# The down projection of layer 2 by rows of tokens: hidden activations stationary, weights moving

## The reference, cut to what matters

```
kv   = einsum('bhsd,bhse->bhde', k, v)
out  = einsum('bhsd,bhde->bhse', q, kv)
x    = (out / rms(out) * g_norm)         # as 4608 x 512
h    = sigmoid(x @ w_gate) * (x @ w_val)     # layer 1, 512 -> 1536
x    = h @ w_out                             # 1536 -> 512
g    = x @ w2_gate
h    = g * sigmoid(g) * (x @ w2_val)         # layer 2
out  = h @ w2_out                            # 4608 x 512, float32
```

## Time and profile before

| | us |
|---|---|
| median of 3 runs | 1740.79 (1740.44 to 1740.86) |
| profiled execution, its own time | 1741.19 |
| its span | 1738.8 |
| PE busy | 1717.6 (99%) |
| DVE busy | 1204.9 (69%) |
| ACT busy | 890.0 (51%) |
| POOL busy | 376.1 (22%) |

### The profile page before, as it was taken

How to read it: one execution, slowest core, us unless ns; L and a number is a source line. 1 busy time by engine, 2 the same in 40 slices (tenths; PEclk the granted TensorE clock), 3 DMA queues, 4 the chain that set the end, 5 groups by cost and what they waited for, 6 DMA issues and landing times.

```text
span 1738.8 us, 30846 instructions
## 1 busy us (share of the span) xinstructions
PE 1717.6 (99%) x11190; PEld 1686.7 (97%) x11190; DVE 1204.9 (69%) x1938; ACT 890.0 (51%) x1709; POOL 376.1 (22%) x326
## 2 busy tenths in 40 slices
PE   8899999999999999999999999999999999999998
PEld 7899999999999999999999999999999999999998
DVE  4876677787666678666679877787666668655556
ACT  5666666555444445444456555555444445444444
POOL 5822222013111125111136000013111124111111
PEclk9999999999999999999999999999999999999999
DMA  9887887586555567555556555576555566555553
GB/s 232 252 264 209 277 254 211 211 298 229 200 200 200 200 222 250 197 198 199 195 188 216 195 198 199 199 250 241 201 198 197 200 220 238 167 180 186 184 187 97
DMA packets 200150, 366.91 MB, mean 211 GB/s; under 512 B 49984, under 2 KB 160064, under 8 KB 200000
## 3 DMA queue, kind: packets, MB, share of 16 engines
q1 hardware_dynamic: 199776, 364.56, 62.8%
q10 hardware_dynamic: 224, 0.39, 0.1%
HBM read 234.36 MB, written 130.55 MB: 210 GB/s over the span
## 4 chain that ended last, share of the span: by engine, by line
PE 93%; DVE 2%; DMA 2%; issue 1%; SPq 0%; POOL 0%; ACT 0%; DVEq 0%; ACTq 0%; POOLq 0%
PE ps L845 87%; PE ps L702 2%; PE ps L687 1%; DMA wops<-in_v_dram 1%; PE ps L692 1%; PE ps L714 1%; PE ps L768 1%; DVE arena L1399 1%; DVE wa L1255 0%; DMA arena<-in_q_dram 0%; DVE arena L1417 0%; DVE xo L1260 0%; PE ps L671 0%; SPq L415 0%; DMA g<-in_g_norm_dram 0%
## 5 line engine op out<-in xcount | busy, mean ns | idle before, releaser
L845 PE MATMUL ps<-xo,wa 128*128 128x384 f32 x6048 | 1076.4, 336 | 4.4 <-DVE arena L1399 1.9
L845 PEld LDWEIGHTS ps<-xo,wa 128*128 128x128 f32 x6048 | 1045.8, 188 | 8.2 <-issue 3.4
L1042 ACT ACTIVATE arena<-ps 128x384 f32<-128x384 f32 x648 | 316.9, 491 | 574.0 <-PE ps L845 572.5
L1399 DVE TENSOR_TENSOR arena<-ps,arena 128x384 f32<-128x384 f32 x648 | 352.3, 553 | 359.0 <-PE ps L845 282.6
L845 PE MATMUL ps<-hop,wb 128*128 128x384 f32 x3024 | 537.9, 335 | 1.2 <-DVE arena L1417 0.9
L845 PEld LDWEIGHTS ps<-hop,wb 128*128 128x128 f32 x3024 | 523.0, 188 | 4.9 <-issue 2.5
L1670 POOL TENSOR_TENSOR arena<-arena 128x384 f32<-128x384 f32 x144 | 146.8, 1045 | 734.9 <-DVE arena L1399 734.9
L1349 DVE TENSOR_TENSOR hop<-arena,hop 128x384 fp32r<-128x384 f32 (+1 forms) x396 | 275.3, 718 | 33.9 <-ACT hop L1024 28.0
L1024 ACT ACTIVATE hop<-arena 128x384 fp32r<-128x384 f32 (+1 forms) x396 | 233.5, 609 | 61.1 <-DVE arena L1417 33.4
L1056 ACT ACTIVATE arena<-arena 128x384 f32<-128x384 f32 x216 | 112.5, 521 | 66.6 <-DVE arena L1399 66.6
L1417 DVE TENSOR_TENSOR arena<-arena 128x384 f32<-128x384 f32 x216 | 129.2, 600 | 20.3 <-DVE arena L1399 1.4
(11 more groups left out here) (75 smaller groups left out, 779.4 us busy)
## 6 DMA issues: line engine op xcount, KB each, us to landing
xo<-x_operands SPq DMA_DIRECT2D x168, 768.0 KB, 6.2
x_operands<-xo SPq DMA_DIRECT2D x84, 768.0 KB, 5.2
x<-arena SPq DMA_DIRECT2D x120, 384.0 KB, 2.9
arena<-x SPq DMA_DIRECT2D x96, 384.0 KB, 4.5
xraw<-x SPq DMA_DIRECT2D x22, 768.0 KB, 6.3
wops<-in_moe_w_gate_dram SPq DMA_DIRECT2D x24, 256.0 KB, 5.1
wops<-in_moe_w_val_dram SPq DMA_DIRECT2D x24, 256.0 KB, 4.5
wops<-in_moe_w_out_dram SPq DMA_DIRECT2D x48, 128.0 KB, 2.3
```

What stands on the lines that cost most here:

```text
L845: mm = pe.matmul(dst, lhsT, rhs, start=(pr in (1, 5, 2) and c == 0 and i == 0), stop=(c == 1 and i == 2), skip_group_check=(pr in (6, 7, 4 ...
L1042: nc.scalar.activation(dst, X(side), ACT.Copy).then_inc(copied, 1)
L1399: nc.vector.tensor_tensor(dst, acc, buf, ALU.add).then_inc(summed, 1)
```

## The change

Layer 2's down window (`by_rows`) swaps the operands. The hidden activations of 128 tokens are stationary, the weights of 256 output features move. Side 0 now holds token chunks 0 and 1 of the three in a half (bank width 512), side 1 chunk 2 (width 256). Copies, totals and GpSimd's additions of this window work on 512 and 256 elements in place of 384 and 384. x2 becomes tokens by features. The turning, its copies and its stages go; the output is stored straight from `res`, in six DMAs for each token half (rows of two runs of 1 KB), by SyncE at the end of the `qq` of the last pass; in the last block ScalarE issues three of the twelve.

```diff
-    x2 = nc.dram_tensor("x2", [DM, N], F32, kind="Internal").ap()
+    x2 = nc.dram_tensor("x2", [N, DM], F32, kind="Internal").ap()
...
+        ROWS = HN // P
+        RH = 2 * P
+        ROW_CHUNKS = ((0, 1), (2,))
+        def by_rows(qq, w):
+            return place(qq)[0] == 1 and w == 2
+        def bank_part(bank, qq, w, side):
+            return ps[:, bank + side, 0:RH * len(ROW_CHUNKS[side]) if by_rows(qq, w) else HN]
+        def buf_part(buf, qq, w, side):
+            if by_rows(qq, w):
+                at = ROW_CHUNKS[side][0] * RH
+                return buf.rearrange("p s n -> p (s n)")[:, at:at + RH * len(ROW_CHUNKS[side])]
+            return buf[:, side]
...
+        def out_rows(qq, t):
+            for k in range(ROWS):
+                at = BLK * place(qq)[2] + HN * t + P * k
+                edge = SP_ - at % SP_
+                for first, n in ((0, edge), (edge, P - edge)):
+                    b, c, row = (at + first) // S, (at + first) % S // SP_, (at + first) % SP_
+                    src = res[:, t].rearrange("p h s n -> p h (s n)")[first:first + n, :, RH * k:RH * (k + 1)]
+                    yield out_dst[b, c, row:row + n].rearrange("r (h d) -> r h d", h=2), src
+        OUT_PIECES = 2 * ROWS
...
             def load_res(qq, t, half):
                 if last_result(qq - 1):
-                    sp.wait_ge(turned, n_turn(qq - 1, HT * t + HT - 1))
+                    sp.wait_ge(out_stored[t], 16 * OUT_PIECES * (qq - (QN - NB)))
...
+            def store_out(qq, t):
+                if t == 1:
+                    sp.wait_ge(part_added, n_part(qq, 22, 1))
+                    sp.wait_ge(c21_done, 2 * qq + 2)
+                else:
+                    sp.wait_ge(part_added, n_part(qq, 11, 1))
+                    if qq < QN - 1:
+                        sp.wait_ge(part_added, n_part(qq, 12, 1))
+                    else:
+                        sp.wait_ge(summed, n_summed(qq, 2, 12, 1))
+                for i, (dst, src) in enumerate(out_rows(qq, t)):
+                    if qq < QN - 1 or t == 1 or i % 2 == 0:
+                        sp.dma_start(dst, src).then_inc(out_stored[t], 16)
...
-            def turn(qq, i):
...
-                for d in range(KC):
-                    mm = pe.transpose(ps[:, 6 + i % 2, d * P:(d + 1) * P], res[:, t, d // 2, d % 2, at:at + P], ident[:])
-                mm.then_inc(turned, 1)
...
-                        for i, (wp, xp) in enumerate(((HI, HI), (HI, LO), (LO, HI))):
+                        if by_rows(qq, w):
+                            for k in ROW_CHUNKS[side]:
+                                for i, (wp, xp) in enumerate(((HI, HI), (HI, LO), (LO, HI))):
+
+                                    mm = pe.matmul(dst[:, k % 2 * RH:(k % 2 + 1) * RH],
+                                                   hop[:, HOP_SLOT[pr], xp, c, k * P:(k + 1) * P],
+                                                   wb[:, c, W_AT[pr], wp, :],
+                                                   start=(pr in (1, 5, 2) and c == 0 and i == 0 and k % 2 == 0),
+                                                   stop=(c == 1 and i == 2), skip_group_check=True)
...
-                        if c == 1 and qq > 0 and last_result(qq - 1) and w == 0 and s in TURN_AT:
-                            turn(qq - 1, TURN_AT[s])
...
-            for i in ENDING:
-                turn_end(i)
...
-                        if turning and w == 0 and s in TURN_AT:
-                            rows(TURN_AT[s])
...
+            act.wait_ge(part_added, n_part(QN - 1, 11, 1))
+            act.wait_ge(summed, n_summed(QN - 1, 2, 12, 1))
+            for i, (dst, src) in enumerate(out_rows(QN - 1, 0)):
+                if i % 2 == 1:
+                    nc.scalar.dma_start(dst, src).then_inc(out_stored[0], 16)
```

More of the change, by code:

```diff
@@ L215, in first_cols @@
             return HN if u < UPB else BLK - S
[L218 to L223, removed]
-        ps = ctx.enter_context(nc.psum_tensor("ps", [P, 8, 512], F32))
+        ROWS = HN // P
+        ps = ctx.enter_context(nc.psum_tensor("ps", [P, 8, 512], F32))
+        RH = 2 * P
[9 more added lines that the diff above has]
+            return buf[:, side]
         def X(side):
             return ps[:, side, 0:HN]
[L230 to L234, removed]
+        X_BANK, W_BANK, Z_BANK = 0, 2, 4
         ident_zero = sem("ident_zero")
@@ L496, in store_res @@
                     sp.wait_ge(part_added, n_part(qq, c, 1))
[L497 to L506, removed]
+                sp.dma_start(res_dram(qq, t, half), res_place(qq, t, half)).then_inc(res_stored[2 * t + half], 16)
+            def store_out(qq, t):
[11 more added lines that the diff above has]
+                        sp.dma_start(dst, src).then_inc(out_stored[t], 16)
             load_unit(0)
@@ L589, in _ @@
                     if turning:
[L590 to L594, removed]
+                        for t in (1, 0):
+                            for half in range(2):
+                                load_res(qq, t, half)
                     if is_late(u):
@@ L655, in _ @@
                     store_res(qq, 12)
[L656 to L660, removed]
-                else:
[L662 to L666, removed]
+                else:
+                    store_out(qq, 1)
+                    store_out(qq, 0)
+            for stored in out_stored:
+                sp.wait_ge(stored, 16 * OUT_PIECES * NB)
         @block.tensor
@@ L1030, in copy @@
                     def copy(pr, side):
[L1031 removed]
+                        dst = buf_part({1: p_buf, 6: u2_buf, 7: u3_buf}[pr], qq, w, side)
                         c = {1: 11, 6: 12, 7: 22}[pr]
@@ L1066, in copy_c21 @@
                             act.wait_ge(res_stored[res_sem(21)], 16 * stored_before(qq))
[L1067 to L1073, removed]
-                                act.wait_ge(stored, 32 * HT * (qq - 1 - (QN - NB)))
-                        nc.scalar.activation(o_stage[i], ps[:, 6 + i % 2, :], ACT.Copy).then_inc(o_copied, 1)
+                        nc.scalar.activation(buf_part(res[:, t, half], qq, w, side), bank_part(X_BANK, qq, w, side), ACT.Copy).then_inc(c21_done, 1)
                     u = late_unit(qq, w)
@@ L1388, in total @@
                             t, half = RES_AT[c]
-                            dst = res[:, t, half, side]
+                            dst = buf_part(res[:, t, half], qq, w, side)
                             if p == 0 and stored_before(qq) > 0:
@@ L1404, in total_21 @@
                         dve.wait_ge(res_loaded[res_sem(21)], 16 * (partial(qq) + 1))
-                        nc.vector.tensor_tensor(res[:, t, half, side], X(side), res[:, t, half, side], ALU.add
-                                                ).then_inc(c21_done, 1)
+                        dst = buf_part(res[:, t, half], qq, w, side)
+                        nc.vector.tensor_tensor(dst, bank_part(X_BANK, qq, w, side), dst, ALU.add).then_inc(c21_done, 1)
                     def hidden(c):
@@ L1660, in _ @@
                         t, half = RES_AT[c]
-                        buf = {11: p_buf, 22: u3_buf, 12: u2_buf}[c][:, side]
-                        dst = res[:, t, half, side]
+                        buf = buf_part({11: p_buf, 22: u3_buf, 12: u2_buf}[c], qq, 2, side)
+                        part = buf_part(res[:, t, half], qq, 2, side)
+                        dst = part
                         if qq == QN - 1 and c == 12:
@@ L1669, in _ @@
                         pool.wait_ge(res_loaded[res_sem(c)], 16 * (partial(qq) + 1))
-                        nc.gpsimd.tensor_tensor(dst, buf, res[:, t, half, side], ALU.add).then_inc(part_added, 1)
+                        nc.gpsimd.tensor_tensor(dst, buf, part, ALU.add).then_inc(part_added, 1)
                     if first_unit is not None:
```

69 lines of the change are left out of this document (14 added, 55 removed).

## The result

The changed kernel takes 1734.49 us (median of 7 runs, 1733.75 to 1736.68), the kernel before beside it 1741.03. The ratio is 0.9961, with a 95% interval of 0.9948 to 0.9974. So it is 6.5 us faster, 0.4% of the time and clear of the noise; forecast were 4.8. The same two kernels timed twice more gave 0.9959 (0.9946 to 0.9972) and 0.9976 (0.9967 to 0.9985): 6.9 and 5.1 us. Every ratio in this document is to the kernel before, timed beside the kernel in question.

A forecast was written before the change was run, and what follows sets the result against it. PE's instruction count times their distance was taken as the bound. Turning -13.7, down windows +9.5 and tail -0.6 sum to -4.8 us: 1741.19 to 1736.4, and 1736.0 for the median; range 1722 to 1751.

The forecast's parts named there:

- PE's own work is the bound: Whole kernel: PE busy 99% at 2.4 GHz and 93% of the span, so time is instruction count times their distance.
- Turning, -13.7: Layer 2's first up windows: removing 24 transposes saves 2.73 us a block, 13.7 us over five blocks.
- The down windows, p = 120.0 ns, +9.5: Layer 2's down windows: 126 matmuls of 256 columns, p apart, replace 84 of 384; 15.12 us each, +9.5 us in sum.
- The comparison with the transposes: PE: transposes start 0.109 us apart against 0.1067 for their columns, so the 13.3 ns extra belongs to fp32r or its load.
- Seventeen windows at 0.56: Layer 2: 17 of 18 down windows end on PE and each grows 0.56 us, +9.5 us; the last counts with the tail.
- The cover holds: Layer 2's down windows: product 7 side 0's copy frees its bank before product 4 needs it, 0.14 us to spare; cost 0.
- Stores and loads: x2 and output DMAs: shorter 1 KB runs and stores queued on SyncE before the `res` loads cost 0.
- The tail, -0.6: From the last down window's start to the span's end: earlier first store saves 0.6 us, with -2 to +1 as ends.
- the floor: Down windows' matmul distance: the weight load is no obstacle until about 0.110 us, giving 13.86 us a window, 0.70 less.
- the first (extra with the columns): Down windows: the extra scales with columns or less, p between 110 and 115.6 ns, 1714.6 to 1726.5 us; chance 24%.
- The second (the load shows): Down windows: weight loads can't hide under 256 columns, p goes towards 173.3 ns, up to +123.8 and 1850 us; chance 15%.
- the even point: Down windows: from a matmul distance of 122.2 ns on, their added time outweighs the 14.3 us gain and the change loses.

## Why the prediction was right

- *PE's own work is the bound.* Right. Each change in the count of PE instructions came back at full size in layer 2: 13.7 for the transposes put back, 9.3 for the form taken away.
- *Turning, -13.7.* Measured -13.6, and the transposes put back alone make 31.86 us of the pair again.
- *The down windows, p = 120.0 ns, +9.5.* The distance was exact, 0.120, and the choice between 115.6 and 120.0 was the one that the sum hung on. The reason given for it, a constant for each matmul or load, holds from 384 to 256 columns but isn't a rule: the extra is 13.3 at four sizes and 14 to 20 at four others. That 256 is one of the four was luck. With the 20.0 of 448 columns each window would have been 0.84 us longer, and the change a loss of some 9 us (an estimate, 17 x 0.84 - 5.2). The comparison with the transposes, from which the extra was laid to this type, proves nothing either: fp32r matmuls of 128 columns start 0.112 us apart, the transposes 0.109, so both may be held by the weight load.
- *Seventeen windows at 0.56.* The step is a little too large: in 13 of 17 places the window and the step behind it grew by about 0.553, but the windows of `qq` 18, 24 and 30 grew by only 0.31 and that of 29 by 0.49. There PE had idle time before (in 24, 14.887 against 14.56), and the longer PE work covered a part of it: in `qq` 24 the wait came behind the first three matmuls and took 0.29 us; now it comes behind six, 0.2 us later in the window, and takes 0.09. The sum was 8.6.
- *The cover holds.* Right, with the spare time worked out as 0.14 and probed as 0.13.
- *Stores and loads.* Right: SyncE waits 4.9 us in all for the output's stores to land before it loads `res` again, and TensorE doesn't pause for any of it (down windows of 15.11 in `qq` 31 to 34, where these stores and loads are).
- *The tail, -0.6.* Measured -0.2. The start was right (first store 15.17 us in, expected 15.0, before 15.90), so 0.7 were gained there. About 0.5 were lost again. The issues were mis-sized: SyncE took 0.6 us for each in the mean, not 0.42. And "same bytes" was not the same work: the DMA engines needed 5.7 us for them in place of 5.1, where the prediction had read from the earlier trace rows that the shorter runs cost nothing. The span's end came 2.3 us after the last issue and not 4.0, so that these errors nearly cancelled, which is luck.
- *The rest.* Forecast -4.8, layer 2 gave -5.2, the medians -6.5, -6.9 and -5.1. What is beyond 5.2 isn't in layer 2. In front of its first down window single profiles scatter by more than that: it starts at 956.9, 960.9 and 957.0 in the kernel before and at 955.9, 954.8 and 956.4 in the changed one. So the median was hit to 1.5 us, and layer 2 to 0.4: 0.9 less cost in the down windows and 0.4 less gain in the tail made up for each other in part.
- *The range.* Half way from 115.6 to the floor (112.8) gives 1720.6 by the prediction's own sum, a little outside its 1722.

Of the rivals, the first (extra with the columns) is refuted by 0.120 and by 512 columns at 0.2269. The second (the load shows) doesn't hold at 256 columns at anything like its full size, though a load of half the columns took 7 ns off there; it becomes true at 224 and below. The change won by little: p of 122.2 was the even point, and the 120.0 are 1.8% under it.

## What to carry to other kernels

Where TensorE is the bound, the columns are only a part of the price: here an fp32r matmul with its weight load cost 13 to 20 ns beside its columns from 256 columns up (12 at 288), and with 128 stationary columns none of the groups came closer than 0.112 us on average. The extra at one size says little of another, so measure the size that you mean to use. So count instructions in both forms: swapping the operands added 42 instructions of 13.3 ns overhead, 0.56 us for a window, three times a block, to save 2.7 us once; by these numbers the gain would be gone at five passes (an estimate, 5 x 0.56 = 2.8). And before a window is shortened between a PSUM bank's release and its next use, work out the spare time of that chain from the copy's row; 0.13 us were left here.

## What the runs showed of the hardware

- fp32r matmuls with a weight load of 128 columns each, at 2.4 GHz: 0.227 us apart for 512 moving columns, 0.217 for 480, 0.207 for 448, 0.188 for 416, 0.173 for 384, 0.161 for 352, 0.147 for 320, 0.120 for 256, 0.112 for 192 and for 128. The amount over the columns is not constant (14.4 ns at 352, 15.0 at 416, 20.0 at 448, 13.6 at 512), which none of the theories foresaw.
- With 128 moving columns, halving the stationary operand to 64 columns brings the matmuls from 0.112 to 0.060 us apart.
- What SyncE needs to issue a store follows the number of rows, not plainly the form of the runs. Medians behind another issue, one run of 2 KB a row (before) against two of 1 KB (after): 64 rows 0.60 and 0.61 us, 96 rows 0.42 and 0.43, 32 rows 0.42 and 0.59 (0.44 where they came second). At the end every issue of the kernel before had 96 rows (0.32 to 0.44), while the nine of the changed kernel are mixed (5.63 together, one of them 0.98).
- 1.57 MB stored in runs of 1 KB kept the DMA engines busy for 5.7 us (5.4 with the issues shared six and six), in runs of 2 KB for 5.1.
- The weight load doesn't hold matmuls of 384 columns: with 32 stationary columns, a quarter of the load, 168 take the same 29.28 us; with 64 and 96 they take a little more (30.00 and 29.56).
